# Attention and two expert layers on one core: last tiles routed in another order, gates inverted in the slots, first loads in halves

## The reference

```python
B, H, S, D = 4, 8, 768, 64                       # N = B * S = 3072 tokens, DM = H * D = 512
scores = (q @ k.T) / sqrt(D)                      # kept: keys 0..3 (sinks) and the 128 keys up to the query
a = softmax(scores);  x = a @ v                   # x: [3072, 512]

logits = x @ w_gate                               # E = 8 experts, F = 1024
e = argmax(logits);  gate = softmax(logits)[e]
x = gate * (max(x @ w1[e], 0) @ w2[e])            # one expert for each token

h = x @ w_in                                      # 512 -> 2048
out = (h - tanh(h)) @ w_out                       # 2048 -> 512
```

## Time and profile before

| | |
|---|---|
| median of 3 runs | 1100.36 us (1098.98 to 1100.69) |
| the profiled execution | 1100.39 us, span 1098.7 us |
| mean granted TensorE clock | 0.997 |
| busy, share of the span | PE 98%, DVE 55%, ACT 44%, POOL 44% |
| DMA | 99.44 MB, mean 91 GB/s |

### The profile page before, as it was taken

One profiled execution on the slowest core, in us unless ns is written; L12 is line 12 of the kernel. 1 busy time (PEld: TensorE's weight loads), 2 busy tenths in 40 slices (PEclk: granted clock), 3 DMA queues, 4 the chain that ended last, 5 costly groups with the idle time before them and its releaser, 6 DMA issues.

```text
span 1098.7 us, 17140 instructions
## 1 busy us (share of the span) xinstructions
PE 1079.1 (98%) x6028; PEld 877.5 (80%) x6028; DVE 609.1 (55%) x1310; ACT 481.7 (44%) x1034; POOL 484.0 (44%) x492
## 2 busy tenths in 40 slices
PE   9999998999999999999999999999999999999997
PEld 6777775788888888888878888888888888888885
DVE  6788785222232223322268766666666666666664
ACT  7888875414233415352354433333333333333332
POOL 3256525707025436484174445335335335334432
PEclk9999999999999999999999999999999999999999
DMA  8646723525115244465222101001011011000000
GB/s 280 201 126 214 260 82 131 182 86 185 55 54 195 89 161 128 143 219 163 68 87 96 51 8 39 20 20 39 10 30 39 1 39 39 1 1 7 33 1 38
DMA packets 37916, 99.44 MB, mean 91 GB/s; under 512 B 8272, under 2 KB 8400, under 8 KB 32720
## 3 DMA queue, kind: packets, MB, share of 16 engines
q1 hardware_dynamic: 29392, 52.30, 15.5%
q0 software_dynamic: 8448, 46.17, 11.9%
HBM read 75.84 MB, written 22.61 MB: 90 GB/s over the span
## 4 chain that ended last, share of the span: by engine, by line
PE 95%; DVE 1%; DMA 1%; issue 1%; ACT 1%; SPq 0%; POOL 0%; POOLq 0%; ACTq 0%; DVEq 0%
PE bank L707 24%; PE bank L715 23%; PE bank L636 15%; PE bank L650 15%; PE bank L452 5%; PE bank L486 4%; PE bank L468 3%; PE bank L642 2%; PE bank L623 1%; PE bank L691 1%; PE bank L530 1%; PE bank L518 1%; PE bank L510 1%; DMA qT<-qt 0%; DMA sorted_x<-x_tok,dest 0%
## 5 line engine op out<-in xcount | busy, mean ns | idle before, releaser
L1444 POOL TENSOR_TENSOR weights<-raw,weights 128x1024 fp32r<-128x1024 f32 x70 | 166.6, 2401 | 201.7 <-ACT weights L775 200.6
L715 PE MATMUL bank<-weights,gT_hi 128*128 128x512 f32 x768 | 238.6, 392 | 0.3 <-DVE gT_lo L1311 0.3
L707 PE MATMUL bank<-mT_hi,weights 128*128 128x512 f32 x768 | 189.8, 389 | 0.7 <-ACT mT_hi L926 0.7
L1538 POOL TENSOR_SCALAR ser<-ser 128x512 f32<-128x512 f32 x96 | 61.8, 644 | 281.5 <-DVE ser L1256 281.4
L707 PEld LDWEIGHTS bank<-mT_hi,weights 128*128 128x128 f32 x768 | 144.1, 188 | 30.8 <-ACT mT_hi L926 0.9
L715 PEld LDWEIGHTS bank<-weights,gT_hi 128*128 128x128 f32 x768 | 142.7, 188 | 29.4 <-DVE gT_lo L1311 0.7
L715 PE MATMUL bank<-weights,gT_lo 128*128 128x512 f32 x384 | 149.6, 390 | 0.0
L650 PE MATMUL bank<-weights,hT_hi 128*128 128x512 f32 x464 | 148.6, 401 | 0.0
L940 ACT ACTIVATE bank<-bank 128x512 f32<-128x512 f32 x96 | 55.9, 582 | 210.7 <-DVE ser L1287 210.7
L636 PE MATMUL bank<-weights,mT_hi 128*128 128x512 f32 x464 | 147.4, 399 | 0.0
L1540 POOL TENSOR_SCALAR sq<-sq 128x512 f32<-128x512 f32 x94 | 140.6, 1496 | 0.0
(11 more groups left out here) (157 smaller groups left out, 1586.4 us busy)
## 6 DMA issues: line engine op xcount, KB each, us to landing
raw<-w_all POOLq DMA_DIRECT2D x32, 1024.0 KB, 5.5
raw<-w_all SPq DMA_DIRECT2D x8, 1024.0 KB, 7.7
sorted_y<-ys SPq DMA_DIRECT2D x30, 257.0 KB, 3.3
xs<-sorted_x SPq DMA_DIRECT2D x29, 257.0 KB, 2.8
kT<-kt SPq DMA_DIRECT2D x24, 264.0 KB, 3.0
qT<-qt SPq DMA_DIRECT2D x24, 256.0 KB, 3.5
v_in<-vt SPq DMA_DIRECT2D x24, 256.0 KB, 3.6
raw<-sorted_y SPq DMA_DIRECT2D x20, 257.0 KB, 2.7
```

Source lines behind the costliest of these rows:

```text
L707: done = e.matmul(bank[HB[n % 3]][:, :], wt[:, f // 2, c, cols], x[:, c, :], start=(m == 0), stop=(m == 3 * CH - 1))
L715: done = e.matmul(bank[YB[i]][:, :], x[:, n % 3, rows], wt[:, f, :], start=(f == 0 and m == 0), stop=(f == GCH - 1 and m == 2))
L1444: e.tensor_tensor(lo, src, hi.bitcast(F32), ALU.subtract).then_inc(s_w_lo, 1)
L1538: e.tensor_scalar(row, row, SERIES_2, 1.0, ALU.mult, ALU.add).then_inc(s_ser, 1)
```

## The change

- **First loads.** SP issues the first tile's keys in two halves, then keys and queries of the second tile, and only then the rest. ScalarE issues the first tile's queries in two halves ahead of its loop. The scores of the first four heads wait for the first halves only.
- **Products on `ones`.** Eight at the start become six, and the four in front of the first transpose become three, one each behind the first and second four scores and between the two first transposes. Later, 32 in front of the first slot become 42, and 11 spare transposes become five.
- **Subtractions.** GpSimd's eight halves are subtracted in the tiles 8 to 12 and 14 to 16.
- **Gates.** The routing leaves the sum of exponentials in the row's gate column. Each slot adds 1e-9 and inverts on VectorE, at the end of its slot body, behind a wait for `load_meta`; `finish` waits for that. For the last three tiles ScalarE writes the sum there itself.
- **Last tiles.** The loops end with the last tile's scores, and what is left is written out on TensorE, ScalarE and VectorE. Tile 22's logits go to another bank and ahead of the last transposes; the last tile's logits are made as tokens by experts at once (`logits_by_token`), without eviction and turn. VectorE reads the ranks of the fourth set ahead of the last `part`.
- **`clear_tail(1)`** stands behind the load of the first slot's rows.
- **First slot.** All products with the high part of `x` come first (`first_up`), and the slot waits for the low part only in front of the ninth product.

```diff
+            if w == ALL - 2:
+                return bank[0]
             return bank[O_BANK] if w == ALL - 1 else bank[R_BANK]
...
+            e.dma_start(kT[:, 0, 0:2, :].rearrange("p a n -> p (a n)"), kt[0, :, 0:2 * HALF]).then_inc(k_first, 16)
+            e.dma_start(kT[:, 0, 2:4, :].rearrange("p a n -> p (a n)"), kt[0, :, 2 * HALF:4 * HALF]).then_inc(k_in[0], 16)
+            load_keys(1)
+            load_queries(1)
             for g in range(ALL):
...
-                e.dma_start(kT[:, g % RING_K, :, :].rearrange("p a n -> p (a n)"), kt[g, :, :]).then_inc(k_in[g % RING_K], 16)
-                e.dma_start(qT[:, g % RING_Q, :, :].rearrange("p a n -> p (a n)"), qt[g, :, :]).then_inc(q_in[g % RING_Q], 16)
+                if g >= 2:
+                    load_keys(g)
+                    load_queries(g)
...
             clear_tail(0)
-            clear_tail(1)
             for b in range(NSETS):
                 e.wait_ge(scattered[b], 16 * SETS[b][1])
...
             load_x()
+            clear_tail(1)
             e.wait_ge(s_loops, 1)
...
-                if p == 0 and g == 0:
-                    keep_warm(4, bk)
...
+            def logits_by_token(w):
+
+                e.wait_ge(s_oT, w + 1)
+                each = P // PAIRS
+                for c in range(PAIRS):
+                    at = R_TURNED.start + c * each
+                    done = e.matmul(logits_bank(w)[:, at:at + 2 * E], oT[:, w % 2, c, :], wg[:, c, 0:2 * E],
+                                    start=True, stop=True, skip_group_check=True)
+                done.then_inc(s_l_turned, 1)
...
-            keep_warm(8)
+            keep_warm(6)
...
-            for i in range(ALL + 3):
+            for i in range(ALL):
...
+                if i == 0:
+                    keep_warm(1, bank[O_BANK])
...
+                if i - 3 in LAST and i < ALL - 1:
+                    rank(LAST.index(i - 3))
+
+            logits(ALL - 2)
+            turn_prob(ALL - 1, 2)
+            turn_prob(ALL - 1, 3)
+            turn_logits(ALL - 2)
+            rank(MULTI - 1)
+            small_bank_read(ALL - 2)
+            turn_sinks(ALL - 1)
+            for p in range(PAIRS):
+                values(ALL - 1, p)
+            rank(MULTI)
+            sink_values(ALL - 1)
+            turn_x(ALL - 2)
+            rank(MULTI + 1)
+            logits_by_token(ALL - 1)
+            turn_x(ALL - 1)
             keep_warm(5, bank[0])
             rank(MULTI + 2)
...
-            keep_warm(32, bank[R_BANK])
+            keep_warm(42, bank[R_BANK])
...
+                def first_up():
+
+                    products = [(xT_hi, wt, c) for c in range(CH) for wt in (w1h, w1l)] + [(xT_lo, w1h, c) for c in range(CH)]
+                    for m, (xp, wt, c) in enumerate(products):
+                        if m < 2 * CH and m % 2 == 0:
+                            e.wait_ge(s_w_lo, c + 1)
+                        if m == 2 * CH:
+                            e.wait_ge(x_split, r["this"])
+                        done = e.matmul(bank[MH[0]][:, :], xp[:, c, :], wt[:, c, 0:512],
+                                        start=(m == 0), stop=(m == 3 * CH - 1))
+                    return done
...
-                e.wait_ge(x_split, r["this"])
-                up(0, range(CH)).then_inc(h_first, 1)
+                if x == 0:
+                    e.wait_ge(x_hi, 1)
+                    first_up().then_inc(h_first, 1)
+                else:
+                    e.wait_ge(x_split, r["this"])
+                    up(0, range(CH)).then_inc(h_first, 1)
...
-            for _ in range(11):
+            for _ in range(5):
                 e.transpose(bank[R_BANK][:, 0:P], ident[:, :], ident[:, :])
...
+            e.dma_start(qT[:, 0, 0:2, :].rearrange("p a n -> p (a n)"), qt[0, :, 0:2 * P]).then_inc(q_first, 16)
+            e.dma_start(qT[:, 0, 2:4, :].rearrange("p a n -> p (a n)"), qt[0, :, 2 * P:4 * P]).then_inc(q_second, 16)
...
+            logits_evict(ALL - 2)
+            part(ALL - 1, 3)
+            sinks_evict(ALL - 1)
+            route_exp(MULTI)
+            route_exp(MULTI + 1)
+            o_evict(ALL - 1)
+            normalise(ALL - 2)
+            route_exp(MULTI + 2)
+            normalise(ALL - 1)
...
-                e.wait_ge(meta_in, r["this16"])
+                e.wait_ge(gate_done, r["this"])
...
-                if b < MULTI:
-                    e.tensor_reduce(gsum[:, 0:tiles], expo[:, 0:tiles], AX_X, ALU.add).then_inc(s_gsum, 1)
-                    yield
-                    e.wait_ge(s_gsum, 2 * b + 1)
-                e.tensor_scalar(gsum[:, 0:tiles], gsum[:, 0:tiles], 1e-9, None, ALU.add).then_inc(s_gsum, 1)
-                yield
-                e.wait_ge(s_gsum, 2 * b + 2 if b < MULTI else MULTI + b + 1)
-                e.reciprocal(gate, gsum[:, 0:tiles]).then_inc(s_gate, 1)
+                e.tensor_reduce(x_tok[:, start % RING_X:start % RING_X + tiles, DM], expo[:, 0:tiles], AX_X,
+                                ALU.add).then_inc(s_gate, 1)
                 yield
...
+            ranks_read = places(MULTI - 1)
+            next(ranks_read)
             part(ALL - 1, 2)
+            at_once(ranks_read)
             at_once(pick(MULTI))
-            at_once(places(MULTI - 1))
-            at_once(gates(MULTI))
-            at_once(places(MULTI))
             invert(ALL - 2)
             add_logits(ALL - 2)
             at_once(pick(MULTI + 1))
-            at_once(gates(MULTI + 1))
+            at_once(places(MULTI))
             invert(ALL - 1)
             at_once(places(MULTI + 1))
             add_logits(ALL - 1)
             at_once(pick(MULTI + 2))
-            at_once(gates(MULTI + 2))
             at_once(places(MULTI + 2))
...
                 lower(hT_lo[:, CH:FCH, :], MHT[1], hT_hi[:, CH:FCH, :]).then_inc(lo_second, 1)
+
+                gate = ys[:, DM:DM + 1]
+                e.wait_ge(meta_in, r["this16"])
+                e.tensor_scalar(gate, gate, 1e-9, None, ALU.add).then_inc(gate_sum, 1)
+                e.wait_ge(gate_sum, r["this"])
+                e.reciprocal(gate, gate).then_inc(gate_done, 1)
...
+            LO_AT = (8, 9, 10, 11, 12, 14, 15, 16)
...
-                if 8 <= i < 16:
-                    split_lo(0, i - 8)
+                if i in LO_AT:
+                    split_lo(0, LO_AT.index(i))
```

More of the change, by code:

```diff
@@ L444, in scores @@
                 if pair == 0:
-                    e.wait_ge(q_in[g % RING_Q], 16 * (g // RING_Q + 1))
-                    e.wait_ge(k_in[g % RING_K], 16 * (g // RING_K + 1))
+                    if g == 0:
+                        e.wait_ge(k_first, 16)
+                        e.wait_ge(q_first, 16)
+                    else:
+                        e.wait_ge(q_in[g % RING_Q], 16 * (g // RING_Q + (1 if g % RING_Q else 0)))
+                        e.wait_ge(k_in[g % RING_K], 16 * (g // RING_K + 1))
+                if pair == 2 and g == 0:
+                    e.wait_ge(k_in[0], 16)
+                    e.wait_ge(q_second, 16)
                 cols = HALF if t == 0 else COLS
@@ L582, in tensor @@
                     turn_sinks(g)
[L583 to L585 removed]
+                scores(i, 2)
+                scores(i, 3)
+                if i == 0:
+                    keep_warm(1, bank[O_BANK])
                 if in_values:
@@ L869, in scalar @@
                     split_hi(0, i - 7)
-            r = {n: e.alloc_register(f"act_{n}") for n in ("this", "next", "this16", "trips")}
+            logits_evict(ALL - 2)
[7 more added lines that the diff above has]
+            normalise(ALL - 1)
+            r = {n: e.alloc_register(f"act_{n}") for n in ("this", "next", "trips")}
             e.wait_ge(s_loops, 1)
@@ L1204, in vector @@
             e.tensor_copy(offs[:, :], sums[:, 1, 3:3 + E]).then_inc(s_offs, 1)
-            r = {n: e.alloc_register(f"dve_{n}") for n in ("this", "next", "trips")}
+            r = {n: e.alloc_register(f"dve_{n}") for n in ("this", "next", "this16", "trips")}
             e.reg_mov(r["this"], 1)
             e.reg_mov(r["next"], 2)
+            e.reg_mov(r["this16"], 16)
             def lower(out_, bk, hi):
@@ L1457, in scatter @@
                 e.wait_ge(s_dest, b + 1)
-                e.wait_ge(s_gate, b + 1)
+                if b < MULTI:
+                    e.wait_ge(s_gate, b + 1)
+                else:
+                    e.wait_ge(s_expo, b + 1)
                 e.wait_ge(s_ids, b + 1)
```

114 lines of the change are left out of this document (56 added, 58 removed).

## The result

The changed kernel takes 1091.93 us in the median of four runs (1091.45 to 1092.35), the kernel before 1099.97 in four runs beside them: a ratio of 0.9927 with a 95% interval of 0.991 to 0.9945. The forecast was 1092.2. The profiled execution took 1091.45 us, its span 1089.7; the profiled one of before had taken 1100.39, so between the two profiles lie 8.94 us, 0.9 more than between the medians.

A forecast was written before the change was run, and what follows sets the result against it. TensorE was taken as the bound, busy 1079.1 of 1098.7 us, with gains only where it waits. Terms 1.7 + 1.3 + 1.4 + 1.5 + 0.1 + 2.2 = 8.2 us off 1100.4 gave 1092.2, range 1089.0 to 1097.4.

The forecast's parts named there:

- First loads, 1.7: At the start, halved first transfers and earlier second-tile loads let scores and queries come sooner: 1.7 us gained.
- Rival 1: At the start, the first loads give nothing, because of ScalarE's table load or busy DMA engines: 1093.9 us; chance 0.20.
- Moved subtraction, 1.3: In attention's 14th tile, VectorE's `v_sink` subtraction no longer takes 1.95 us beside GpSimd's subtraction, but 0.68: 1.3 us gained.
- gates, 1.4: In attention's routing, removing gate operations lets VectorE reach the next maximum 0.7 us earlier, twice: 1.4 us gained.
- Rival 5: In attention, what the change frees is taken up by the same tile's next wait: 1096.4 us; chance 0.09.
- Last tiles, 1.5: At attention's end, a ladder of estimated step times puts the last scatter at 184.8 against 186.46: 1.5 us gained.
- Rival 4: At attention's end, the new order gives nothing, ScalarE's eviction or GpSimd's 0.80 coming later: 1093.7 us; chance 0.14.
- Zeros, 0.1: Moving `clear_tail(1)` gains up to 0.8 on the last scatter and loses up to 0.7 on the load: 0.1 us gained.
- First slot, 2.2: In the first expert slot, earlier products and TensorE kept at its higher clock: 2.2 us gained.
- rival 2: In the first slot, TensorE is at its lower clock again, the gap exceeding 0.7 us: 1093.4 us; chance 0.17.
- The slots' gates, nothing: In the expert slots, the added gate operations cost nothing, since VectorE idles before the next slot's ReLU.
- Rival 3: In the slots, GpSimd's subtractions hold the gate's add and delay the next ReLU: 58 us slower, 1150; chance 0.03.

The follow-up runs named there:

- the last group of runs: Four edits to the changed kernel: 28 products on ones, 1098.35 us; first slot's old order, 1099.92; late gate, 1168.24; last normalisation on VectorE with 36 products, 1097.85.

## Why the prediction was right

**First loads, 1.7.** The size is right in the profile (1.67), and by the term's own step: the queries land when TensorE has come there (0.17 us of waiting). But the term put 0.65 on an earlier start, and what the halves are for was missed. The start itself gained 0.23 us at the first maximum (4.96 to 4.73), since the first scores, behind six products in place of eight, ran at TensorE's slow pace: 1.24 us in place of 0.72. The halves mostly prevent the gap with which TensorE stays at that pace: without them the new order lost 0.9 us against before in the profiled run. That the gap is the cause rests on three traces with one, all slow beyond 10 us, and ten without, none of them; no run varied the gap alone. The term holds less firmly than its size says: of nine further traces with the same start two lost some 0.4 us against before, and one gained 0.9. Rival 1 falls in the profile: the table load stands behind the issues, and the busy DMA engines do not keep the queries from landing earlier.

**Moved subtraction, 1.3, and gates, 1.4.** Right to 0.04 us, each by the step the prediction named. Undone, the subtraction's step comes back whole (8.41), and the addition alone brings back 0.45 of the gates' 0.71. The "scores are late next" is seen as well: after the changed gates VectorE waits 0.81 us for them ahead of the next maximum, at 62.94. Rival 5 falls: the chain carries each saving to the end of attention unchanged.

**Last tiles, 1.5.** The last scatter lies at 184.3 on the clock of before, where 184.8 was predicted. The term was under-sized by 0.66, of which 0.16 was taken off the ladder's 1.66 for a queue of waits, and 0.5 lies in the ladder itself. Its first half is right (the sinks' turn waits 0.32 instead of 1.24). Its small VectorE steps up to the last `pick` that ScalarE waits for were put too long: the last output eviction begins at 174.60, which is 178.95 on the clock of before, where the ladder has 179.5; from its end to the scatter it takes 4.75 us against the 4.7 of the ladder. In the old order 0.33 comes from the fourth set's gate operations, which the term did not count. Rival 4, nothing, falls.

**Zeros, 0.1.** The step that failed is the balance of a gain and a loss. The second write does hold up the last scatter's landing (5.15 us with two, 3.93 with one, beside each other); a loss of the load beside it there was none, 2.7 us either way. The gain is not kept whole because of the 42 products: their end was put 0.7 ahead of the rows, and it lies some 0.6 behind them.

**First slot, 2.2.** Right in kind, 0.3 too high. The clock stayed at 1.00, and rival 2 falls. The first stage ends 4.18 us after the transposes begin, not 4.0: the first product stands 1.33 behind them, as put, but the twelve take 2.85 and not 2.7. And before it ended 6.07 after them, not 6.2: twelve products from 196.62 to 200.34 are 3.72, not 3.8. The difference is the 1.89.

**The slots' gates, nothing.** Right: the chain runs through TensorE in every slot, and its stages past the first slot take as long as before. In seven slots the addition waited for the slot's `meta`, up to 3.2 us, and that stayed under the cover. (The slowest `meta` before landed 3.4 us behind the median, 5.1 against 1.7, not 3.5.) Rival 3 stays unfulfilled: an operation on one number a row is not held. Why is not shown. The Trainium skill, VectorE: DVE Perf Modes, section "What auto-detection actually checks", says that an operation takes the mode 2×_2P, a two-port mode, if a single source and the destination are in SBUF and their outermost dimensions other than one are both even or equal. A row of six numbers has such a dimension and a row of one has none, so that would explain it, and both durations agree with it.

The median, 1091.93, is nearer to the forecast than the profile's own sum (8.94 against 8.2), and that is luck: the errors of +0.7, +0.6 and -0.3 add up to 1.0, the terms as traced come to 0.9 over the forecast, and the profiled execution of the changed kernel happens to be the fastest of its four.

## What to carry to other kernels

A saving in a wait is kept when the next late thing is named and measured, as with the scores behind the gates; then steps of the chain give each term to a tenth of a microsecond. Work that only keeps TensorE busy must end when the real operands come: too little leaves a gap, too much becomes the path itself. And where an early load decides whether TensorE pauses, splitting it can be worth more than its bytes; but leave a margin, since here 0.1 us of pause went with a loss of 2 us in two traces.

## What was not expected

TensorE's pace at the start: after a pause of 0.66 us, and of 0.11 and 0.14, it stays at about half until past 10 us, with 1.00 in the column of the granted clock; products of 0.61 to 0.63 us instead of 0.39 show it. Without a pause it rises at 3.9 to 6.5 us, not at the same time in each trace.

In the last group of runs all four variants had ScalarE stand still ahead of the last tile's eviction for 2.58 to 3.30 us, ended by something outside the core's engines ("remote"), though the products that it evicts had ended. At 90 to 92.5 us VectorE had stood still for 3.3 us and ScalarE for 1.0, ended by the same, and in the tail ScalarE took up the logits of the tile before only after 0.75 to 0.78 us of idling, though their products took 0.43 us as ever. A 20 KB packet on the queue named "instruction" lies at the start of that pause, and also in the undisturbed traces, where nothing pauses. Late instruction loads would fit, but no run here separates that from other causes: this group ran on another chip than the two groups before it, and the changed kernel itself was not run beside it.
